# A chunked attention and expert kernel: three sums of squares, one exponential, six weight loads and some filler matmuls change place

## The reference, cut to what matters

```python
mag = np.sqrt(a_re * a_re + a_im * a_im)
scale = np.minimum(mag, 0.999) / (mag + 1e-06)
a_re_n, a_im_n = (a_re * scale, a_im * scale)
for t in range(S):                       # B, H, S, D = 4, 8, 768, 48
    new_re = ar * S_re - ai * S_im
    new_im = ar * S_im + ai * S_re
    S_re, S_im = (new_re + kv, new_im)   # kv = outer(k[t], v[t])
    y[:, :, t] = np.einsum('bhd,bhde->bhe', q[:, :, t], S_re)
...
logits = x @ phi                         # x = y, 3072 tokens x 384
...                                      # softmax over tokens, 8 experts, softmax over 32 slots
return (h * h @ w_out).astype(np.float32)   # h = relu(x @ w_in), 384 -> 2048 -> 384
```

## Time and profile before

| | |
|---|---|
| median of 3 runs | 657.55 us (654.57 to 658.29) |
| the profiled execution | 659.17 us, its span 657.4 us |
| PE busy | 515.7 us (78%), 4537 matmuls |
| DVE busy | 406.3 us (62%) |
| ACT busy | 351.9 us (54%) |
| POOL busy | 138.8 us (21%) |
| DMA | 79.59 MB, mean 121 GB/s |
| chain that ended last | PE 55%, DVE 17%, DMA 10%, ACT 9%, SyncE's queue 4% |

### The profile page before, as it was taken

One profiled execution on the slowest core, in us unless ns is written; L12 is line 12 of the kernel. 1 busy time (PEld: TensorE's weight loads), 2 busy tenths in 40 slices (PEclk: granted clock), 3 DMA queues, 4 the chain that ended last, 5 costly groups with the idle time before them and its releaser, 6 DMA issues.

```text
span 657.4 us, 11676 instructions
## 1 busy us (share of the span) xinstructions
PE 515.7 (78%) x4537; PEld 390.3 (59%) x4537; DVE 406.3 (62%) x660; ACT 351.9 (54%) x592; POOL 138.8 (21%) x120
## 2 busy tenths in 40 slices
PE   1000256896859969898499986999999999999997
PEld 1000045674636746676388752458888888888886
DVE  4699995899978999997454214159842333233322
ACT  5575706379428793337333431167665656565653
POOL 7000000000000000000000000027655555555553
PEclk9999978798869997999799999999999999999999
DMA  6120074662675526779689899900010101010001
GB/s 255 47 98 0 18 161 160 132 133 56 192 156 118 125 55 132 209 219 232 150 173 218 246 420 427 408 4 0 1 49 0 49 0 49 1 49 1 14 35 48
DMA packets 40023, 79.59 MB, mean 121 GB/s; under 512 B 7200, under 2 KB 28832, under 8 KB 38048
## 3 DMA queue, kind: packets, MB, share of 16 engines
q1 hardware_dynamic: 36224, 62.33, 33.7%
q10 hardware_dynamic: 3744, 16.52, 7.8%
HBM read 55.12 MB, written 4.72 MB: 91 GB/s over the span
## 4 chain that ended last, share of the span: by engine, by line
PE 55%; DVE 17%; DMA 10%; ACT 9%; SPq 4%; issue 4%; ACTq 0%; DVEq 0%
PE ps L1304 10%; PE ps L1301 9%; PE ps L1300 9%; DMA stk<-xout 7%; PE ps L1034 7%; SPq L263 4%; PE ps L1274 3%; DMA big<-in_a_all 3%; PE ps L1020 3%; DVE xout L830 2%; DVE tt L741 2%; PE ps L1194 2%; PE ps L1074 2%; PE ps L1216 2%; PE ps L1077 2%
## 5 line engine op out<-in xcount | busy, mean ns | idle before, releaser
L999 DVE TENSOR_TENSOR qs<-rs 128x512 f32<-128x512 f32 x96 | 83.0, 865 | 118.5 <-ACT rs L615 118.5
L678 POOL TENSOR_TENSOR hlo<-qs,hhi 128x512 fp32r<-128x512 f32 x96 | 126.3, 1315 | 131.0 <-DVE qs L999 127.5
L1020 PE MATMUL ps<-ident 128*32 128x512 bf16 x245 | 73.5, 403 | 61.3 <-DVE xout L830 61.3
L1034 PE MATMUL ps<-stk 112*128 112x224 f32 (+1 forms) x384 | 87.1, 387 | 37.9 <-DMA stk<-xout 37.9
L1300 PE MATMUL ps<-hhi,who 128*128 128x512 f32 x285 | 110.9, 389 | 0.0
L1301 PE MATMUL ps<-hhi,wlo 128*128 128x512 f32 x285 | 110.9, 389 | 0.0
L1034 PEld LDWEIGHTS ps<-stk 112*128 112x128 f32 x384 | 76.5, 217 | 50.8 <-DMA stk<-xout 45.1
L615 ACT ACTIVATE rs<-ps 128x512 f32<-128x512 f32 x96 | 57.4, 598 | 82.3 <-PE ps L1274 82.1
L1304 PE MATMUL ps<-hlo,who 128*128 128x512 f32 x285 | 80.5, 391 | 0.1
L670 POOL MEMSET sinz<- 128x768 f32 x1 | 0.7, 739 | 370.8 <-PE ps L1077 370.8
L1020 PEld LDWEIGHTS ps<-ident 128*32 128x32 bf16 x245 | 19.8, 99 | 82.4 <-DVE xout L830 61.6
(11 more groups left out here) (160 smaller groups left out, 816.4 us busy)
## 6 DMA issues: line engine op xcount, KB each, us to landing
stk<-xout SPq DMA_DIRECT2D x144, 128.0 KB, 3.8
wt<-in_w SPq DMA_DIRECT2D x10, 1536.0 KB, 17.2
xq<-in_xq SPq DMA_DIRECT2D x24, 384.0 KB, 4.6
big<-in_a_all ACTq DMA_DIRECT2D x9, 768.0 KB, 7.6
vr<-in_v_all SPq DMA_DIRECT2D x24, 192.0 KB, 5.0
wt<-in_w ACTq DMA_DIRECT2D x3, 1536.0 KB, 9.5
wt<-in_w ACTq DMA_DIRECT2D x6, 768.0 KB, 6.6
out<-ost SPq DMA_DIRECT2D x5, 768.0 KB, 3.5
```

The source lines that it names most:

```text
L678: pool.tensor_tensor(hlo[:, i % NHS, :], qs[:, i % NQS, :], hhi[:, i % NHS, :].bitcast(F32), ALU.subtract).then_inc(lo_ready, 1)
L999: dve.tensor_tensor(qs[:, i % NQS, :], rs[:, i % NQS, :], rs[:, i % NQS, :], ALU.mult).then_inc(sq_ready, 1)
L1020: nc.tensor.matmul(ps[P - SL:P, bank, :], idb[:, 0:SL], idle, start=True, stop=True)
L1034: last = nc.tensor.matmul(ps[:, h // 2, h % 2 * SK:h % 2 * SK + cols], x[:, 0:CH], x[:, CH:CH + cols], start=True, stop=True)
```

## The change

Six edits, in the hand-written lists:

- ScalarE takes the raw squares of tiles 1 and 2 (c = 1) behind `copy_kt` and behind `copy_state` of that chunk, where all three tiles stood ahead of `copy_kt`. VectorE's three `norm2` move from the end of c = 1 to three places in c = 2.
- The exponential is cut in two: chunk 0's columns (384) before the sign planes, the other chunks' (1920) behind them. `weigh` of chunk 0 waits for the first, of the others for the second.
- In stage 3 the first squares of the products (L404) move ahead of `exponentials`, and the last of them ahead of `copy_y`.
- In stage 4 `load_half` moves from the head of each chunk behind its `copy_kt`.
- TensorE runs 20 filler matmuls where there were 10 before `scores(0)`.
- It runs 20 where there was 1 before `scores(18)`.

```diff
                 act.wait_ge(m_log, 2 * (b + 1))
-                m = grid(M_[b % 2], [1, PF])
-                nc.scalar.activation(m, m, ACT.Exp, scale=-1.0).then_inc(m_ready, 1)
+                exponential(b, 0, 1)
+
+            def exponential(b, c, count):
+                x = grid(M_[b % 2] + 2 * c, [HP, TF], [2 * NC, HC // 2], [1, 2 * count])
+                nc.scalar.activation(x, x, ACT.Exp, scale=-1.0).then_inc(m_ready, 1)
...
-                    if p == B and c < NC:
-                        if c == 0:
-                            act.wait_ge(chain, C_ALL * B)
-                            act.wait_ge(kq_ready, 2 * NC * (B - 1))
-                        load_half(NC + c)
                     if p < B - 1:
                         prepare(p + 1, c, 0)
-                        if c in (1, NC - 2):
+                        if c == NC - 2:
                             prepare(p + 1, c, 1)
                             prepare(p + 1, c, 2)
+                    if p == B - 1 and c == NC - 2:
+                        product_squares(p, 0, 0)
+                        product_squares(p, 0, 1)
...
                         copy_kt(n, 1)
+                    if p == B and c < NC:
+                        if c == 0:
+                            act.wait_ge(chain, C_ALL * B)
+                            act.wait_ge(kq_ready, 2 * NC * (B - 1))
+                        load_half(NC + c)
...
-                    if p < B - 1 and 2 <= c < NC - 2:
+                    if p < B - 1 and 1 <= c < NC - 2:
                         prepare(p + 1, c, 1)
                     if p < B and c == NC - 2:
-                        product_squares(p, 0, 0)
-                        product_squares(p, 0, 1)
+                        product_squares(p, int(p == B - 1), 0)
+                        product_squares(p, int(p == B - 1), 1)
...
                     if c == NC - 1 and p < B - 1:
                         signs(p + 1)
+                    if c == NC - 1 and p < B:
+                        exponential(p, 1, NC - 1)
...
-                    if p < B - 1 and 2 <= c < NC - 2:
+                    if p < B - 1 and 1 <= c < NC - 2:
                         prepare(p + 1, c, 2)
-                    if p < B and c == NC - 2:
+                    if p < B - 1 and c == NC - 2:
                         product_squares(p, 1, 0)
...
-                dve.wait_ge(m_ready, b + 1)
+                dve.wait_ge(m_ready, 2 * b + 1 + (c > 0))
...
+                    if p < B - 1 and c == 2:
+                        norm2(p + 1, 0)
                     if p < B:
                         parts_in(p, lo, mid)
+                    if p < B - 1 and c == 2:
+                        norm2(p + 1, 1)
...
                         parts_in(p, mid, hi)
-                    if p < B - 1 and c == 1:
-                        for t in range(DT):
-                            norm2(p + 1, t)
+                    if p < B - 1 and c == 2:
+                        norm2(p + 1, 2)
...
-            keep_busy(10)
+            keep_busy(20)
...
-                        keep_busy(6 if full else 1)
+                        keep_busy(20 if n == NT - NC else 6 if full else 1)
```

## The result

The changed kernel takes 646.27 us (median of 4, 645.81 to 648.25) against 657.33 (median of 4, 654.57 to 658.29). The ratio is 0.9842, with a 95% interval of 0.9811 to 0.9873: 11 us faster, where 10.8 was forecast. The profiled execution went from 659.17 to 645.81 us and its span from 657.4 to 644.1, so it moved 13.4, more than the medians did.

A forecast was written before the change was run, and what follows sets the result against it. It saw the kernel bound by VectorE's waits at sums and batch ends, and slow scores behind restacks. Its running sum went -2.0, -5.4, -7.0, -11.8, then +1.0 for the tail: -10.8, 646.8 us median, range 640 to 653.

The forecast's parts named there:

- the likeliest course: The forecast itself over the whole kernel: 10.8 us faster, 646.8 us for the median; chance 0.40.
- Fillers before `scores(0)`: Chunk 0: twenty fillers make the scores take 3.29 us instead of 6.25; raw loads issued near 90, not a gain.
- Restacks 1 and 7: Chunks 1 and 7: restacks beside raw loads take 14.0 and 13.0 us; `scores(1)` at 104.0, `scores(7)` taken at 184.2.
- between these two the restack loses 1.63 us for each us that the loads come sooner: Restacks 1 and 7: a line between 9.2 us (loads 2.95 behind the restack's issue) and 15.3 (0.81 ahead).
- A head start buys nothing: Rival at restacks 1 and 7: each restack beside raw loads takes 15.3 us, whichever came first; 649.3 us, chance 0.20.
- share evenly: DMA queues at the restacks: two transfers in flight share evenly, whoever was first by some tenths; step behind the 15.3 us.
- Sums one chunk later: Batch 2, chunks 2 and 3: 0.4 of 6.8 us idle time comes back, 1.6 more at the masks; -2.0 in all.
- Signs before the rest of the exponential: Batch ends: signs about 1.6 us sooner, VectorE's 1.36 us wait before `init_products(2)` goes, -3.4 in all there.
- Stage 3's squares: Stage 3: squares end sooner, but the logarithm waits for the copies of `logits(15)`; nothing gained unless those come sooner.
- Half load and fillers at chunk 18: Chunk 18: restack 18 takes 2.5 us less without the half load, its scores 2.3 us less; together -11.8 so far.
- they delay nothing: Chunk 18: the 19 new fillers need at most 4.2 us, and about 5 us stay after the last logits.
- The tail: Behind the attention: half loads come later, some where DMA engines are full; +1.0 us, bounds none and 3.9.

The follow-up runs named there:

- one piece: The changed kernel with the inverse squares' exponential in one piece ahead of the signs; ratio 0.9953 against the kernel before.
- ten fillers: The changed kernel with ten fillers instead of twenty ahead of the scores of chunk 0; ratio 0.9769 against the kernel before.
- weights late: The changed kernel with raw loads and the third batch's three loads of experts' weights behind the copy of the state; ratio 0.9662 against the kernel before.
- the late loads: Runs of the changed kernel with the three raw loads issued behind the copy of the state; ratio 0.9688 with only that changed.
- late raw loads: The changed kernel with the three raw loads behind the copy of the state, not the second copy of the scores; ratio 0.9688 against the kernel before.
- fourteen fillers: The changed kernel with fourteen fillers instead of twenty ahead of the scores of chunk 18; ratio 0.9851 against the kernel before.
- ten fillers and late raw loads: The changed kernel with ten fillers ahead of the scores of chunk 0 and raw loads behind the copy of the state; ratio 0.9682 against the kernel before.

## Why the prediction was right, point by point

The sum was right, 10.8 against 11, and up to chunk 18 the likeliest course was the one that happened. That the total came so near is partly luck. The sum was made for the profiled execution, and the profiles moved by 13.4; up to the end of `scores(18)` they moved 10.0 where 11.8 was forecast, and behind it they gained where a loss was forecast. The medians moved less than the profiles because the old profile is 1.8 us above its median and the new one 0.5 below.

**Fillers before `scores(0)`: right.** They took 6.51 us and ended at 85.03, the scores took 3.29, the raw loads were issued at 90.46, "at 90.0". That this is "not a gain" was too mild. Undone, it is worth 4.8 us, with an error of 3.6.

**Restacks 1 and 7: the step that failed is "between these two the restack loses 1.63 us for each us that the loads come sooner".** Two points were taken for a line. The fourteen profiles give the curve. Lag is from the restack's first issue to the first raw load's, time is from that issue to the scores:

| lag, us | time of restack 1 or 7, us | seen in |
|---|---|---|
| -0.8 | 15.3, 15.4 | before, one piece |
| 0.2 to 0.3 | 14.8 to 15.5 | changed, and five experiments |
| 0.6 to 1.2 | 14.4 to 16.0 | changed, and four experiments |
| 1.4 to 1.9 | 13.1 to 13.8 | five experiments |
| 3.0 | 9.2 | before |
| 3.3 to 3.4 | 7.2 | ten fillers; weights late |
| 3.9 to 5.1 | 7.1 to 8.1 | the late loads |

(Where TensorE comes late itself, the time is an upper bound.) It is flat at 15 up to a lag of a microsecond, and from (1.2, 14.9) to (3.3, 7.2) it falls by 3.6 us per us, until the restack is as fast as alone (7.1). For chunk 1 the line gave 14.0, and it was 15.5; for chunk 7 it gave 13.0, the text took 184.2 for the scores, and they came at 185.59. Up to a lag of 1.2 us this is what the rival *A head start buys nothing* said, and its 15.3 fits the 14.4 to 16.0.

Why the curve has this form is seen in what the two queues moved. From 94 to 98 us of the changed kernel both are in flight (packets, MB, share of the 16 engines' time):

```profile
q10 hardware_dynamic: 335, 0.97, 80.9%
q1 hardware_dynamic: 260, 0.25, 22.9%
```

q10 has the raw loads and q1 SyncE's DMAs, the restack first. They don't share evenly: the raw loads get over three times the engines' time and four times the bytes. From 102 to 106 us the loads are all but through, and q1 has 100.8%. The same is seen around restack 7, 78.3% against 23.6% from 175 to 180 us. So what counts is how much of its 0.79 MB the restack has moved before the loads are under way. From 90 to 94 us q1 moved 0.13 MB in the changed kernel (lag 0.27), 0.39 with late raw loads (1.72) and 0.64 with ten fillers (3.31). The rule that the rival leant on (the Trainium skill, DMA: Bandwidth & Descriptors, Queues, rings and completion order) is a round robin between the queues, a packet at a time. In packets the trace agrees roughly, 335 to 260. But a packet of the raw loads has 2.9 KB on average and one of q1 has 1.0, so the prediction's "share evenly" does not follow from it; that step was wrong, though its 15.3 came out.

**Sums one chunk later: right in its mechanism, optimistic in sign.** "So of the 6.8 us of idle time this place gives back only 0.4": it gave back nothing (119.99 against 119.17, with the start 0.35 later), and alone it costs 2.7. The 1.6 for the masks' wait behind `scores(2)` came back as forecast, since these now run in 3.29 us: counted from the first keys, chunk 4's come 1.2 us sooner than before. Chunk 5's come another 0.9 sooner, which no term had, and so the stage ended with the forecast -2.0 (2.07 found at chunk 6's keys). "For batch 1 the same move costs nothing" wasn't tried apart.

**Signs before the rest of the exponential: the placing right, the total mis-sized.** 3.4 forecast at `init_products(2)`, 3.2 found; 242 forecast for `init_products(3)`, 242.63 found; `weigh(18)` near 309, 309.19 found. The three ends add to 1.5 + 1.6 + 1.8, near what the terms say. But undone alone the part is worth 7.3 us, since a late VectorE also meets other waits, in chunk 16 among them, where it makes matmuls slow as well.

**Stage 3's squares: right**, worth nothing that can be measured.

**Half load and fillers at chunk 18: right in the profile, the coupling missed.** -2.5 and -2.3 were added as if they were separate. The start came 7.7 sooner (forecast: 7.0 + 2.5) and the end 10.0 (forecast: 11.8), because the landing at about 318 was not what the scores waited for: the fillers ran until 319.4. The step "they delay nothing" failed: it set the fillers against the wait as it was, with the last logits ahead of the restack. `weigh(18)` and restack 18 came 6.7 us sooner, but `scores(17)`, which wait 13.8 us for a restack of their own (with the last weight load issued 1.5 ahead of it), only 3.6 (310.96 to 307.39). So `turn_x` and the logits behind them start 3.1 us after restack 18's first issue, where they started 1.1 ahead of it, and the fillers stand behind the logits. With fourteen fillers those 1.4 us are seen to come back, and in that profile to be lost in the tail.

**The tail: wrong in sign, and open.** +1.0 was forecast; this profile's stretch from chunk 23's keys to the last matmul on experts' weights fell from 65.1 to 62.3 us. The wait that was to grow is the 5.72 us of the earlier trace rows, which the prediction took for one for the weights (the row says only `issue`). It shrank (start us, us, what, in the chain that ended last):

```profile
396.91 1.96 issue
398.87 2.78 PE ps L1207 x24
```

Behind the longer wait the same 24 matmuls took 4.08 us (410.91 to 414.99, with a granted clock of 0.74 from 411 to 416 us), so it cost clock as well. The prediction's price rested on the half loads that move into the tail, but the tail gained. The twelve experiments give 62.1 to 65.2 with no pattern that I can name, and with the half load at its old place it is 64.5. From there to the end of the span all fourteen profiles take 231.3 or 231.4 us: "its own length unchanged" was right.

So the parts, each by its undoing: exponential 7.3, half load 5.5, fillers at 18 1.7, squares 1.2, sums -2.7, fillers at 0 -4.8. They sum to 8.2 of the 10.4 us that the ratio of 0.9842 makes; each has an error of 2.3 to 3.6 us, so those of 1.7 and 1.2 can't be told from nothing, and some of them act together.

## What to carry to other kernels

Before an engine or an edit makes a transfer start sooner, look at what is in flight on the other queue at that moment: here 3 us of faster matmuls cost 8 us of restack, and loads issued 1.5 and 4 us later gained 10. Two points of a collision are not a line; vary the lag and look for the flat part and the edge. And when one change holds six edits, undo each: the first of them gained nothing, one cost 4.8 us, and three load issues moved by a few lines were worth as much again as all six together.

## What the runs showed of the hardware

The time of a small transfer (six DMAs of 128 KB) beside a large one (three of 768 KB, on another queue) depends on the lag: about 15 us up to a lag of 1.2 us, 7 to 8 from 3.3 on, and a steep slope between. While both are in flight the large one, with packets of 2.9 KB against 1.0, has 80.9% of the engines' time against 22.9%.

The clock under the same filler matmuls differs from one profiled execution to the next, where the programs are the same up to there. Twenty fillers took 5.89, 6.07 and 6.51 to 7.14 us, and the shorter they were, the more of `scores(0)` ran slowly: 4.98 us after 5.89 and 6.07, 3.29 after 6.51 and more. The pause before the scores was 2.65 and 2.60 us in the first two, and at most 2.09 in the others. No length of the pause divides them everywhere: at chunk 18 one of 2.34 left the scores at 3.29, `scores(2)` took 3.29 behind 2.66 (ten fillers) and 2.83 (ten fillers and late raw loads), and `scores(3)` took 4.97 behind 2.23 (late raw loads). The Trainium skill (TensorE: Matmul & The Clock Gate, Part 1) says that the number of slow matmuls at a start varies from run to run of one kernel; the 5.89 to 7.14 fit that, though no kernel here was profiled twice. Since the raw loads hang on these scores, slower scores move the lag: from 0.2 or 0.3 to 1.8 us with the loads where the change has them (13.3 instead of 15 us), and from 1.7 to 3.4 with them behind the state's copy (7.2 instead of 13.4). Whether this is what divides the executions of one kernel wasn't seen, since each was profiled once.
